# Slot weights of a soft mixture: 24 gathers become 31 scatters and one load, and second matrices arrive in halves

## The reference

```python
# 1: gated recurrent attention, 4 batches x 8 heads x 768 steps, head dim 40 -> x: 3072 tokens x 320
# 2: mixture of experts, one expert of 8 for each token
logits = x @ w_gate; e = argmax(logits); g = softmax(logits)[e]
x = g * (relu(x @ w1[e]) @ w2[e])            # w1: 320 x 1024, w2: 1024 x 320
# 3: soft mixture, 8 experts x 4 slots = 32 slots
logits = x @ phi                             # 3072 x 32
d = softmax over tokens(logits)
slot_input = d.T @ x                         # 32 x 320
slot_out[e] = relu(slot_input[e] @ v1[e]) @ v2[e]   # 4 slots for each of 8 experts
c = softmax over slots(logits)               # 3072 x 32
out = c @ slot_out                           # 3072 x 320
```

## Time and profile before

| | us |
|---|---|
| median of 3 runs | 650.33 (647.69 to 654.19) |
| profiled execution | 648.21 |
| its span, first to last instruction | 646.5 |
| TensorE busy in the span | 557.5 (86%), 3643 matmuls |
| VectorE / ScalarE / GpSimd busy | 376.2 / 251.8 / 313.7 |
| mean granted TensorE clock | 0.914 |
| moved by DMA | 91.63 MB, mean 142 GB/s |

### The profile page before, as it was taken

One profiled execution on the slowest core, in us unless ns is written; L12 is line 12 of the kernel. 1 busy time (PEld: TensorE's weight loads), 2 busy tenths in 40 slices (PEclk: granted clock), 3 DMA queues, 4 the chain that ended last, 5 costly groups with the idle time before them and its releaser, 6 DMA issues.

```text
span 646.5 us, 12037 instructions
## 1 busy us (share of the span) xinstructions
PE 557.5 (86%) x3643; PEld 478.8 (74%) x3644; DVE 376.2 (58%) x656; ACT 251.8 (39%) x606; POOL 313.7 (49%) x241
## 2 busy tenths in 40 slices
PE   2899998999999317999999999999999999886583
PEld 1798997998898316898888888989889889822022
DVE  6488886798689693644737767474654334330013
ACT  3776765866574521223323233233233233210003
POOL 3455553655364444554899668593570000107600
PEclk9998996998699555999999999999999999979588
DMA  8999999999992002335451505050501800199047
GB/s 115 160 198 223 199 236 223 207 245 229 208 244 53 20 2 71 97 109 171 134 165 47 201 22 191 21 191 21 185 12 39 330 12 1 33 342 286 19 163 244
DMA packets 149689, 91.63 MB, mean 142 GB/s; under 512 B 108128, under 2 KB 142944, under 8 KB 145568
## 3 DMA queue, kind: packets, MB, share of 16 engines
q1 hardware_dynamic: 138784, 80.58, 51.4%
q0 software_dynamic: 2256, 5.48, 3.4%
q10 hardware_dynamic: 8624, 5.26, 2.6%
HBM read 78.07 MB, written 8.47 MB: 134 GB/s over the span
## 4 chain that ended last, share of the span: by engine, by line
PE 46%; SPq 15%; DVE 13%; DMA 12%; issue 8%; POOL 3%; ACT 2%; DVEq 0%; POOLq 0%; ACTq 0%
DMA ys<-x_tokens,slot_i 7%; PE bank L1288 5%; PE bank L1290 5%; PE bank L1289 5%; SPq L347 4%; SPq L348 4%; PE bank L1271 4%; PE bank L1417 3%; PE bank L1273 3%; PE bank L1272 3%; PE bank L1299 3%; PE bank L1193 2%; SPq L361 2%; DVE gates L1002 2%; PE bank L1313 2%
## 5 line engine op out<-in xcount | busy, mean ns | idle before, releaser
L556 POOL TENSOR_TENSOR W_low<-W,W_high 128x3072 fp32r<-128x3072 f32 (+1 forms) x14 | 87.2, 6228 | 7.2 <-ACT W_high L694 6.3
L1288 PE MATMUL bank<-W_high,h_high 128*128 x248 | 79.3, 320 | 1.5 <-DVE h_low L1027 1.4
L740 ACT ACTIVATE h_high<-bank 128x512 fp32r<-128x512 f32 x62 | 33.7, 595 | 119.6 <-PE bank L1299 115.4
L593 POOL TENSOR_TENSOR W_high<-W,ones 128x3072 fp32r<-128x3072 f32 (+1 forms) x12 | 58.6, 4883 | 37.5 <-PE bank L1290 37.5
L1289 PE MATMUL bank<-W_high,h_low 128*128 x248 | 76.6, 309 | 0.0
L1290 PE MATMUL bank<-W_low,h_high 128*128 x248 | 76.5, 309 | 0.0
L623 ACT ACTIVATE arena<-arena 128x128 f32<-128x128 f32 x192 | 60.6, 391 | 17.4 <-DMA arena<-log_decays 12.8
L1271 PE MATMUL bank<-W_high,x_high 128*128 x124 | 52.9, 427 | 5.7 <-DVE x_high L1010 2.5
L983 DVE TENSOR_TENSOR yc<-bank,slot_gate 128x320 f32<-128x320 f32 x31 | 15.2, 492 | 72.9 <-PE bank L1290 72.9
L1015 DVE TENSOR_SCALAR hb<-bank 128x512 f32<-128x512 f32 x31 | 21.3, 689 | 56.8 <-PE bank L1275 56.8
L1002 DVE TENSOR_TENSOR gates<-gates,rmx (+1 forms) x31 | 52.0, 1681 | 0.0
(11 more groups left out here) (235 smaller groups left out, 1268.9 us busy)
## 6 DMA issues: line engine op xcount, KB each, us to landing
W<-in_moe_w_rows_dram SPq DMA_DIRECT2D x13, 1280.0 KB, 8.4
W<-in_moe_w_main_dram SPq DMA_DIRECT2D x13, 1024.0 KB, 5.2
arena<-log_decays SPq DMA_DIRECT2D x24, 512.0 KB, 5.2
W<-in_moe_w_rest_dram SPq DMA_DIRECT2D x21, 256.0 KB, 5.9
xs<-ys ACTq DMA_DIRECT2D x29, 160.0 KB
ys<-in_q_dram SPq DMA_DIRECT2D x24, 160.0 KB, 5.1
ys<-in_k_dram SPq DMA_DIRECT2D x24, 160.0 KB, 5.7
ys<-in_v_dram SPq DMA_DIRECT2D x24, 160.0 KB, 5.2
```

The lines of the kernel that those rows point to most:

```text
L556: g.tensor_tensor(W_low[:, w], W[:, w], W_high[:, columns(e % 2, part_)].bitcast(F32), ALU.subtract).then_inc(w_split[part_], 1)
L593: g.tensor_tensor(W_high[:, columns(e % 2, part_)], w, ones[:, 0:1].broadcast_to(list(w.shape)), ALU.mult).then_inc(high_ready, 1)
L1288: mm(dst, h_high[:, kk, :], high, start=(kk == 0), stop=False)
```

## The change

It does these things.

1. x_dram has token p of tile t in row p*24 + t. The store writes with that stride (a row of 1,280 bytes per partition, 30,720 bytes apart), and token_tile and token_row are made so that slot_tok names such rows.
2. c_dram is in token order too, with 31*128 rows more behind it. back_i is, for each sorted place, the row p*24 + t of its token, or a row of its own in the part behind (no_token) where the place is empty. DVE makes it with three instructions more (slot_row, back, back_i), POOL has one iota more.
3. ACT's combine_exp only takes the exponential; the last two tiles are taken one by one. POOL scatters each sorted tile to c_dram with an indirect DMA, 31 in all. These stand behind the last weight split and ahead of the memsets.
4. POOL's 24 gathers are gone. ACT, behind its last exponentials and ahead of soft_steps(0), waits for all scatters (c_stored) and loads ctok with one DMA, 3,072 consecutive bytes per partition.
5. PE's transpose_combine stands ahead of soft1(1) and not behind it.
6. All soft experts' v2 come in two DMAs of 640 KB instead of one of 1,280 KB, each with a semaphore. soft2 waits for the first halves of its four experts ahead of kk = 0 and for the second halves ahead of kk = 4. For experts 6 and 7 the order is 6 first half, 7 first half, 6 second half, 7 second half.

```diff
@@ -63,9 +63,9 @@
     TILES = NT + E - 1
     assert (B, C, NP, G4, E, NF) == (4, 6, 4, 4, 8, 8) and SLOTS == 32 and DM == H * D
 
-    x_dram = nc.dram_tensor("x_tokens", (NT * P, DM), F32).ap()
+    x_dram = nc.dram_tensor("x_tokens", (P * NT, DM), F32).ap()
     g_dram = nc.dram_tensor("log_decays", (BH, S), F32).ap()
-    c_dram = nc.dram_tensor("combine_slots", (TILES * P, SLOTS), F32).ap()
+    c_dram = nc.dram_tensor("combine_slots", (P * NT + P * TILES, SLOTS), F32).ap()
 
     with ExitStack() as ctx:
         offset_of = {}
@@ -182,6 +182,10 @@
         slot_tok = sb("slot_tok", [P, TILES])
         slot_gate = sb("slot_gate", [P, TILES])
         slot_i = sb("slot_i", [P, TILES], I32)
+        slot_row = sb("slot_row", [P, TILES])
+        back = sb("back", [P, TILES])
+        back_i = sb("back_i", [P, TILES], I32)
+        no_token = sb("no_token", [P, TILES])
         pen = sb("pen", [P, TILES])
 
         hb = sb("hb", [P, F])
@@ -272,7 +276,7 @@
         small_in = sem("small_in")
         tile_in = [sem(f"tile_in{n}") for n in range(3)]
         weights_in = sem("weights_in")
-        soft_in = [[sem(f"soft_w1_in{n}"), sem(f"soft_w2_in{n}")] for n in range(E)]
+        soft_in = [[sem(f"soft_w1_in{n}"), sem(f"soft_w2a_in{n}"), sem(f"soft_w2b_in{n}")] for n in range(E)]
         dve_chain = sem("dve_chain")
         g_scan = sem("g_scan")
         g_exp = sem("g_exp")
@@ -313,6 +317,7 @@
         e_in, e_exp, c_in, c_exp = sem("e_in"), sem("e_exp"), sem("c_in"), sem("c_exp")
         sl_sum, sl_done, sin_ready = sem("sl_sum"), sem("sl_done"), sem("sin_ready")
         c_max, c_stored, c_back, c_sums = sem("c_max"), sem("c_stored"), sem("c_back"), sem("c_sums")
+        back_ready = sem("back_ready")
         e_sum, sin_tr, sin_scaled = sem("e_sum"), sem("sin_tr"), sem("sin_scaled")
         soft_h, soft_relu = sem("soft_h"), [sem("soft_relu0"), sem("soft_relu1")]
         so_ready = sem("so_ready")
@@ -357,7 +362,8 @@
 
             def store(t, n):
                 sp.wait_ge(x_ready, t + 1)
-                dst = x_dram[ds(t * P, P), :] if dynamic(t) else x_dram[t * P:(t + 1) * P, :]
+                dst = x_dram.rearrange("(p t) d -> p t d", t=NT)
+                dst = (dst[:, ds(t, 1), :] if dynamic(t) else dst[:, t:t + 1, :]).rearrange("p a d -> p (a d)")
                 sp.dma_start(dst, xs[n][:, 0:DM]).then_inc(x_stored[n], 16)
 
             def load_expert(e, slot, n, parts=(0, 1, 2)):
@@ -384,8 +390,10 @@
                 sp.dma_start(raw[:, 0:2 * F], v1_main[e]).then_inc(there, 16)
                 sp.dma_start(raw[0:KD[2][1], 2 * F:W1N], v1_rest[e]).then_inc(there, 16)
 
-            def load_soft_w2(e):
-                sp.dma_start(soft_place(e)[:, W1N:WN], v2[e]).then_inc(soft_in[e][1], 16)
+            def load_soft_w2(e, halves=(0, 1)):
+                for x in halves:
+                    a, z = x * W2N // 2, (x + 1) * W2N // 2
+                    sp.dma_start(soft_place(e)[:, W1N + a:W1N + z], v2[e][:, a:z]).then_inc(soft_in[e][1 + x], 16)
 
             def load_soft(e):
                 load_soft_w1(e)
@@ -440,8 +448,9 @@
             load_soft_w1(6)
             load_soft_w1(7)
             sp.wait_ge(soft_done, 1)
-            load_soft_w2(6)
-            load_soft_w2(7)
+            for x in range(2):
+                load_soft_w2(6, (x,))
+                load_soft_w2(7, (x,))
             fin = ys[:, 0:NT * DM].rearrange("p (t d) -> p t d", d=DM)
             for a, z in OUT_PARTS:
                 for n in range(2):
@@ -536,8 +545,9 @@
                                     base=0, pattern=[[1, P]], channel_multiplier=-1))
             g.iota(col_iota[:, :], pattern=[[1, P]], base=0, channel_multiplier=0, allow_small_or_imprecise_dtypes=True)
             ch.step(g.iota(tile_iota[:, :], pattern=[[P, 32]], base=0, channel_multiplier=0, allow_small_or_imprecise_dtypes=True))
-            g.iota(token_tile[:, :], pattern=[[P, NT]], base=0, channel_multiplier=0, allow_small_or_imprecise_dtypes=True)
-            g.iota(token_row[:, :], pattern=[[0, 1]], base=1, channel_multiplier=1, allow_small_or_imprecise_dtypes=True)
+            g.iota(token_tile[:, :], pattern=[[1, NT]], base=1, channel_multiplier=0, allow_small_or_imprecise_dtypes=True)
+            g.iota(token_row[:, :], pattern=[[0, 1]], base=0, channel_multiplier=NT, allow_small_or_imprecise_dtypes=True)
+            g.iota(no_token[:, :], pattern=[[P, TILES]], base=P * NT, channel_multiplier=1, allow_small_or_imprecise_dtypes=True)
             g.memset(keep[:, :, :], 1.0)
 
             ch.step(g.memset(tile_iota[:, 0:1], -1.0))
@@ -594,6 +604,12 @@
                                     ALU.mult).then_inc(high_ready, 1)
                     split_low(e, part_)
 
+            pool.wait_ge(back_ready, 1)
+            for j in range(TILES):
+                pool.wait_ge(c_exp, j + 1)
+                g.indirect_dma_start(c_dram, bass.IndirectOffsetOnAxis(ap=back_i[:, j:j + 1], axis=0),
+                                     cexp[:, j, :], None).then_inc(c_stored, 16)
+
             pool.wait_ge(tiles_done, TILES + 1)
             for n in range(QUADS):
                 g.memset(hs[n], 0.0).then_inc(hs_clear, 1)
@@ -601,10 +617,6 @@
             for r in range(4):
                 g.tensor_copy(spread[:, r, :, :, :], ident[:, :].rearrange("p (i x s) -> p x i s", i=GRP, s=PER)[:, 0:2, :, :]).then_inc(spread_ready, 1)
 
-            pool.wait_ge(c_stored, 16 * (TILES - 1))
-            for t in range(NT):
-                g.indirect_dma_start(ctok[:, t, :], None, c_dram,
-                                     bass.IndirectOffsetOnAxis(ap=pos_i[:, t:t + 1], axis=0)).then_inc(c_back, 16)
 
 
         @block.scalar
@@ -718,14 +730,11 @@
                 dst = ys[:, ds(j * DM, DM)] if dynamic(j) else ys[:, j * DM:(j + 1) * DM]
                 s.activation(dst, yc[:, 0:DM], ACT.Copy).then_inc(y_kept, 1)
 
-            def combine_exp(j, n=1):
+            def combine_exp(j):
 
                 act.wait_ge(c_in, j + 1)
-                x = cexp[:, ds(j, 1), :] if dynamic(j) else cexp[:, j:j + n, :]
+                x = cexp[:, ds(j, 1), :] if dynamic(j) else cexp[:, j:j + 1, :]
                 s.activation(x, x, ACT.Exp).then_inc(c_exp, 1)
-                act.wait_ge(c_exp, j + 1)
-                dst = c_dram[ds(j * P, P), :] if dynamic(j) else c_dram[j * P:(j + n) * P, :]
-                act.dma_start(dst.rearrange("(j p) s -> p j s", p=P), x).then_inc(c_stored, 16)
 
             def expert_step(j, n, jj, first=False, last=False):
 
@@ -760,7 +769,11 @@
             for n, (a, z) in enumerate(E_PARTS):
                 act.wait_ge(e_in, n + 1)
                 s.activation(et[:, a:z, :], et[:, a:z, :], ACT.Exp).then_inc(e_exp, 1)
-            combine_exp(TILES - 2, 2)
+            combine_exp(TILES - 2)
+            combine_exp(TILES - 1)
+            act.wait_ge(c_stored, 16 * TILES)
+            act.dma_start(ctok, c_dram[0:P * NT, :].rearrange("(p t) s -> p t s", t=NT)).then_inc(c_back, 16)
+
             def soft_steps(q):
 
                 act.wait_ge(soft_h, 2 * q + 1)
@@ -967,11 +980,16 @@
             ch.step(v_.tensor_copy(slot_tok[:, :], tok[:, 0, :]))
             ch.step(v_.tensor_tensor(slot_tok[:, :], slot_tok[:, :], tok[:, 1, :], ALU.add))
 
+            v_.tensor_scalar(slot_row[:, :], slot_tok[:, :], -1.0, 0.0, ALU.add, ALU.max)
             ch.step(v_.tensor_scalar(slot_i[:, :], slot_tok[:, :], -1.0, 0.0, ALU.add, ALU.max))
             dve.sem_inc(routed, 1)
             dve.wait_ge(r_gates_high, 1)
             v_.tensor_tensor(gate_parts[:, :, 1, :], gate_hot, gate_parts[:, :, 0, :].bitcast(F32), ALU.subtract).then_inc(r_gates_split, 1)
             ch.step(v_.tensor_scalar(pen[:, :], slot_tok[:, :], 1.0, -1.0, ALU.min, ALU.add))
+            ch.step(v_.tensor_tensor(back[:, :], pen[:, :], no_token[:, :], ALU.mult))
+            ch.step(v_.scalar_tensor_tensor(out=back_i[:, :], in0=back[:, :], scalar=-1.0, in1=slot_row[:, :],
+                                            op0=ALU.mult, op1=ALU.add))
+            dve.sem_inc(back_ready, 1)
             ch.step(v_.tensor_scalar(pen[:, :], pen[:, :], -NEG, None, ALU.mult))
 
             def y_scale(j):
@@ -1086,7 +1104,7 @@
 
             for q in range(QUADS):
                 if q == 1:
-                    dve.wait_ge(c_back, 16 * NT)
+                    dve.wait_ge(c_back, 16)
                     ch.step(v_.tensor_reduce(rinv[:, :], ctok, AX.X, ALU.add))
                     ch.step(v_.tensor_scalar(rinv[:, :], rinv[:, :], EPS, None, ALU.add))
                     v_.reciprocal(rinv[:, :], rinv[:, :]).then_inc(c_sums, 1)
@@ -1429,9 +1447,10 @@
 
             def soft2(q):
                 pe.wait_ge(hs_ready, 2 * q + 2)
-                for e in range(GRP * q, GRP * (q + 1)):
-                    pe.wait_ge(soft_in[e][1], 16)
                 for kk in range(NF):
+                    if kk % (NF // 2) == 0:
```

(6 more changed lines are left out.)

## The result

The changed kernel took 652.73 us in the median of 20 executions (648.21 to 657.66), the kernel before 650.46 beside it (20 executions, 646.39 to 656.86). The ratio is 1.0048, with a 95% interval of 1.0026 to 1.0071. I had said 635.1, and faster by over 1% with a chance of 0.72. The time lies outside the range too. Executions of one kernel fall into a faster and a slower state; ratios and intervals here use the faster ones alone, and a ratio is not the quotient of the two medians given beside it.

What follows compares the result with a forecast made beforehand. It took POOL's 24 gathers to hold TensorE back from about 589 to 616 us. Gains 13.2 + 1.7 + 0.5 - 0.2 = 15.2 us gave a median of 635.1 us, range 625 to 650.

Steps and rivals of the forecast that it cites:

- (1): POOL's 31 scatters replace the 24 gathers; 21 go back to back in 26 us from 481.7; cost on the path nothing.
- third rival: The scatters take the slow pace with them into the expert stage: 666 us, chance 0.14.
- first rival: Something other than the gathers slows TensorE from 589 to 616 us, so the slow pace stays: 648.3 us, chance 0.13.
- (2): ACT's wait for all scatters and ctok load before soft1's relu: first soft2 up to 1.9 us later, no cost in the sum.
- second rival: ACT's two landings in a row, store and load, take 16.4 us each and delay the second soft1: 640 us, chance 0.13.
- (3): Second soft1 still starts at 600.8 us, waiting for experts 6 and 7's first matrices; gain zero to 3 us, taken as zero.
- (4): Second soft1, for experts 4 to 7, takes 7.9 us, starting at half clock, and ends at 608.7: gain 13.2 us.
- (5): Weight transposes and ACT's copy move into the wait before the second soft1, so soft2 follows 1.8 us behind: gain 1.7 us.
- (6): Second matrices of experts 6 and 7 are there before soft2 wants them, whole or halved: gain 0.
- (7): Expert stage, where ACT no longer issues a store per tile: gain between 0 and 2 us, taken as 0.5.
- (8): Routing, with a few more instructions and x_tokens rows 30,720 bytes apart: cost 0.2 us, between 0 and 1.

Runs made afterwards that it cites:

- fourth set: Control, scatters spread and scatters limited to two under way, run side by side where TensorE is held; the kernel before takes 648.36 us.
- second and fifth sets: Two sets of follow-up runs, each with the kernel before traced again; it takes 649.44 us in the second and 647.88 us in the fifth.
- control: The changed kernel with one register instruction more, masking PE's expert number; 631.64 us (0.9875) with TensorE undisturbed, 650.33 (1.0005) and 652.6 us (1.0042) with it held.
- warming: Seven unread matmuls ahead of the second soft1, added to the control: 648.72 us, 1.0016; added to the spread scatters: 632.52 us, 0.988.
- spread version: Control with its scatters spread, six in a row and then three with each tile: 630.55 us (0.9847) and, where TensorE is held, 632.91 us (0.9751).
- first and third sets: Two sets of follow-up runs in which the kernels with scatters weren't held; the kernel before takes 640.44 us and 639.18 us.
- plain stores: Changed kernel with POOL storing each tile's weights by plain DMA instead of indirect scatter, in sorted order, without bringing into token order: 627.03 us, 0.9713.
- two under way: Control with each scatter waiting until the one before the last has landed: 631.99 us (0.9882), 632.6 us (0.9879), and 643.14 us (0.9877) where TensorE is held.
- one under way: Control with each scatter waiting until the one before it has landed: 640.06 us (1.0) and 642.7 us (1.0034).

## Why the prediction was wrong, point by point

- **(1) is the step that failed.** "Cost on the path: nothing" for the scatters. Where TensorE is held, they cost 20 to 22 us of the stage's pace (21.1, 21.7, 20.3), and 652.6 - 632.9 = 19.7 us in the medians of the fourth set. The rest of the change brings 15.5 there, so the train takes all of it and 4.2 more. The timing of the step was right (back to back for 26 us, then one a tile); the load of them on TensorE was put at nothing, though the section on what bounds the kernel had named it for the gathers. By what means a train holds TensorE stays open.
- **The third rival** (the slow pace goes with the scatters) is what happened, at 0.14. Its point of decision was right: from 19 us of slow pace the gain is eaten. Its size was too large (666) by the 10 us of the single scatters, which did no harm. The 21 us for the train alone were met (20.3 to 21.7), in part by luck: the hold spared the first 7 us of the train and ran on 4 us behind it, and it was denser than 0.8 a us (21.1 us of pace in the 22.2 us from 496.2 to 518.4, the low clock behind it included). The 7 us could be read before: the gathers' slow pace began as late.
- What I set against that rival, that spaced gathers do no harm, was right as a fact and wrong as an argument: these scatters weren't spaced.
- **The first rival** (the slow pace isn't of the gathers) fell. With the gathers gone, the first soft2 takes 612.8 to 617.3 us and SP gets its signal at once, while in the kernel before SP gets it 4.3 to 4.6 us behind the end of the last gather in all three traces (615.88, and 611.48 and 616.83 in the second and fifth sets).
- **(2) and the second rival.** The landings are not late where it matters. The last scatter is off POOL at 599.7, ACT issues its load at 605.27 (5.5 us, where I took 11.7 and 6.7 as the low end), and its relu at 608.07 waits for PE, not for the load. No trace parts a landing into queueing and write receipt, so the 11.7 us speak for the late receipt that I named only in being long.
- **(3)** 600.8 was forecast for the second soft1 and 597.73 measured in the undisturbed control. The 3 us are not what I had bounded with "up to 3": the load is no faster (12.1 us, 11.4 before). I had misread, where soft1 starts 4.42 us of "issue" behind the landing at 596.39 (chain, before):

```profile
584.99 11.40 DMA W<-in_moe_w_rest_dram
```

Every kernel with scatters has 0.25 us there, so the other 4.2 go with the hold. The load lands 11.2 to 17.9 us after its issue, from run to run, and it sets this start.
- **(4)** 7.9 us forecast; 7.1, 7.5, 8.1, 10.0, 10.1 measured without warming, between the bounds given. **(5)** soft2 follows soft1 within 1.8 us, as said. **(6)** gain 0: nothing measurable. **(7)** From slot_i to the first soft1 it is 330.3 us in the undisturbed control and 330.8 before. That the difference is the 0.5 us forecast is luck: five other kernels with scatters and no hole, which differ up to there in the spacing of the scatters alone, take 330.8 to 334.2. **(8)** within the scatter of the start (242.6 to 253.0 us).
- The sum, undisturbed: soft1 597.7 to 607.8, soft2 at 609.65, span 630.7, against 600.8, 608.7, 610.5 and 631. Two errors cancel in it: the start 3.1 us early, the half clock 2.2 us longer. The spread version, with the train's cost taken out, gains 15.5 us over the kernel before in the fourth set; 15.2 was the sum. Where nothing is held the control gains only 8.8 (631.6 against 640.4), since the kernel before is faster there too.

## What to carry to other kernels

A cost seen beside a resource that others merely sit next to (here a train of indirect DMAs and TensorE's signals) moves with the resource. When a change takes such a train off one stage, price it in the stage it is moved to, before anything else, and start from the price it had. Then space it: a wait on the progress of the consumer (three scatters a tile) cost nothing and was worth 19.7 us, while a wait on each DMA's own landing cost the whole gain in the tail (1.0 and 1.0034). The spread version beats the kernel before in both kinds of set: 0.9751 where TensorE is held, 0.9847 where it isn't. It beats the changed kernel where TensorE is held; where it isn't, the two (0.9847 and 0.9875, of different sets) are not told apart.

## What the runs showed of the hardware that I had not expected

- The same program, the control, took 631.6, 650.3 and 652.6 us in three sets, while the kernel before went from 640.4 to 649.4 and 648.4. The difference is the hold. It needs both the dense train and something outside of the program that differs from set to set. What that is stays open: on one chip both kinds were met. Every execution, the timed ones too, was recorded by the profiler, and the traces differ in how many of DMA's signals they hold: 4,971 to 4,992 in the first and third sets for kernels with scatters, 4,378 to 4,823 in all other sets, the spread and the plain stores among them. So those sets differ even where no hole is seen. What is missing goes with the train: of the 496 signals of the 31 scatters the traces hold all in the undisturbed control, 237, 232 and 235 where it or the changed kernel is held, 346 in the spread version of the fourth set, and all 496 again for the plain stores of the fifth. I can't exclude that the recording takes part in the hold; a run without the profiler would tell.
- What is left of the kernel before's loss where nothing is held (640.4 against 631.6) wasn't traced and stays open.
- A limit of two under way hardly thins a train when a landing takes 2.1 us (the median with one under way): one each 1.45 us instead of 1.26.
- TensorE, after a wait, does the same 48 matmuls in 5.71 us at its full clock and in 10.1 us at a mean of 0.54. Warming it gave the full clock where TensorE waited 0.3 us between the last unread matmul and soft1 (5.71 us), and not where it waited 6.3 us (7.38); in neither set did the time tell the warmed kernel from the other.
